# Three small moves at the start of a fused attention, MLP and soft-routing kernel: a side product, one load, one scan

## The reference, cut to what matters

```
# 1: recurrent attention, batch 4, 8 heads, 768 steps, head size 48
for t in range(768):
    y[t]  = r[t] @ (state + (u * k[t]) v[t]^T)
    state = w[t] * state + k[t] v[t]^T
# 2: MLP, 3072 tokens, 384 -> 2048 -> 384
h = x @ w_in;  g = h * clip(h + 3, 0, 6) / 6;  x = g @ w_out
# 3: soft routing, 32 slots (8 experts of 4), 3072 tokens
logits = x @ phi
d = softmax over tokens;  slots = d^T x;  slots = relu(slots @ w1[e]) @ w2[e]
out = softmax over slots(logits) @ slots
```

## Time and profile before

| | us |
|---|---|
| time, median of 3 runs (lowest, highest) | 431.91 (431.82, 432.13) |
| the profiled execution's own time | 432.12 |
| its span, first to last instruction | 430.4 |
| PE busy | 410.6 (95%) |
| DVE busy | 333.8 (78%) |
| POOL busy | 196.4 (46%) |
| ACT busy | 155.4 (36%) |

### The profile page before, as it was taken

One profiled execution on the slowest core, in us unless ns is written; L12 is line 12 of the kernel. 1 busy time (PEld: TensorE's weight loads), 2 busy tenths in 40 slices (PEclk: granted clock), 3 DMA queues, 4 the chain that ended last, 5 costly groups with the idle time before them and its releaser, 6 DMA issues.

```text
span 430.4 us, 9672 instructions
## 1 busy us (share of the span) xinstructions
PE 410.6 (95%) x3898; PEld 222.6 (52%) x3898; DVE 333.8 (78%) x535; ACT 155.4 (36%) x263; POOL 196.4 (46%) x183
## 2 busy tenths in 40 slices
PE   8999899999999999999999999989999999999981
PEld 3875555556555555555565555455554443433430
DVE  7798799998988989889889889898866687641142
ACT  2265355533334244144342342432333234211142
POOL 7747888874645663455654456634630012010000
PEclk9999999999999999999999999999999999999996
DMA  8996312468034223403440332131008961589829
GB/s 248 354 392 250 121 60 63 121 244 283 17 111 121 72 55 116 123 0 121 121 121 2 121 119 86 44 113 56 2 0 339 404 216 70 225 319 423 354 83 357
DMA packets 15245, 69.35 MB, mean 161 GB/s; under 512 B 2016, under 2 KB 2656, under 8 KB 13152
## 3 DMA queue, kind: packets, MB, share of 16 engines
q1 hardware_dynamic: 15200, 68.73, 45.0%
HBM read 64.00 MB, written 4.72 MB: 160 GB/s over the span
## 4 chain that ended last, share of the span: by engine, by line
PE 74%; DVE 8%; issue 6%; DMA 5%; POOL 3%; ACT 2%; SPq 0%; POOLq 0%; DVEq 0%
PE hid L544 13%; PE hid L546 12%; PE hid L545 12%; PE l_ps L579 5%; PE y_ps L510 5%; PE l_ps L611 4%; PE sc_ps L445 4%; DMA att<-rkT_dram 3%; PE hid L757 2%; PE inc_ps L470 2%; PE y_ps L527 2%; DVE att L817 2%; PE sc_ps L611 1%; PE hid L738 1%; PE sc_ps L738 1%
## 5 line engine op out<-in xcount | busy, mean ns | idle before, releaser
L1184 ACT ACTIVATE relu<-hid,three 128x512 f32<-128x512 f32 x96 | 65.9, 687 | 141.7 <-PE hid L546 140.9
L544 PE MATMUL hid<-x_split,w_split 128*128 128x512 f16 x288 | 109.4, 380 | 0.0
L546 PE MATMUL hid<-x_split,w_split 128*128 128x512 f16 x288 | 109.1, 379 | 0.0
L545 PE MATMUL hid<-x_split,w_split 128*128 128x512 f16 x288 | 109.1, 379 | 0.0
L904 DVE SCALAR_TENSOR_TENSOR gated<-relu,hid 128x512 f32<-128x512 f32 x96 | 65.1, 679 | 28.3 <-ACT relu L1184 27.7
L914 DVE STREAM_TRANSPOSE ring<-gated 128x512 f32<-128x512 f32 x96 | 68.3, 711 | 3.3
L1332 POOL TENSOR_TENSOR att<-att 128x1024 f16<-128x1024 f32 x20 | 40.5, 2026 | 50.6 <-ACT att L1129 50.6
L1350 POOL TENSOR_TENSOR att<-att 112x512 f32<-112x512 f32 x19 | 22.4, 1181 | 58.7 <-DVE att L829 58.7
L544 PEld LDWEIGHTS hid<-x_split,w_split 128*128 128x128 f16 x288 | 28.2, 98 | 37.5 <-issue 8.6
L546 PEld LDWEIGHTS hid<-x_split,w_split 128*128 128x128 f16 x288 | 28.1, 98 | 34.0
L545 PEld LDWEIGHTS hid<-x_split,w_split 128*128 128x128 f16 x288 | 28.2, 98 | 25.1 <-issue 0.3
(11 more groups left out here) (228 smaller groups left out, 752.5 us busy)
## 6 DMA issues: line engine op xcount, KB each, us to landing
att<-nat_dram SPq DMA_DIRECT2D x20, 576.0 KB, 4.1
att<-rkT_dram SPq DMA_DIRECT2D x22, 448.0 KB, 5.5
att<-w_dram SPq DMA_DIRECT2D x5, 1536.0 KB, 14.2
att<-wT_dram SPq DMA_DIRECT2D x22, 226.2 KB, 4.8
out_dram<-w_split SPq DMA_DIRECT2D x12, 384.0 KB, 3.9
stage<-w_in_dram SPq DMA_DIRECT2D x2, 1536.0 KB, 13.5
ring<-w_outT_dram SPq DMA_DIRECT2D x1, 3072.0 KB, 15.7
stage<-w_dram SPq DMA_DIRECT2D x2, 1536.0 KB, 9.9
```

The lines of the kernel that those rows point to most:

```text
L544: pe.matmul(hid[s % 2][:], high, x_high, start=(q == 0), stop=False)
L545: pe.matmul(hid[s % 2][:], high, x_low, start=False, stop=False)
L546: last = pe.matmul(hid[s % 2][:], low, x_high, start=False, stop=(q == KT - 1))
L1184: nc.scalar.activation(relu_tile(s), hid[s % 2][:], ACT.Relu, bias=three[:], scale=GATE / H_SCALE)\
```

## The change

Four edits. The load of w_outT is issued in front of the load of unit 4's r, k and v rows (`load_nat(4)`). In unit 3 two of the three parts of w_out times phi replace three `stay_warm` matmuls, two ahead of `attend_first(3)` and one behind it; the third part takes the place of the first in MLP step 0, and the parts in steps 1 and 2 are gone. On DVE the low half of piece 1 goes behind the prefix scan of unit 5 (the sixth unit), and the transpose into w_phi goes from step 4 to step 1.

```diff
             sp.dma_start(u_all, u.rearrange("h d -> (h d)").partition_broadcast(P)).then_inc(u_in, 16)
+            sp.dma_start(w_outT_stage, w_outT).then_inc(w_outT_in, 16)
             load_nat(B)
-            sp.dma_start(w_outT_stage, w_outT).then_inc(w_outT_in, 16)
             load_rows(B + 1)
...
                     turn_keys(n)
-                stay_warm(2, hid[0])
+                if n + 1 < B:
+                    stay_warm(2, hid[0])
+                else:
+                    weigh_phi(0)
                 attend_first(n)
                 if n + 1 < B:
                     diagonal(n + 1)
-                stay_warm(1, hid[0])
+                    stay_warm(1, hid[0])
+                else:
+                    weigh_phi(1)
                 turn_x(n)
...
                 if s == 0:
                     turn_keys(B)
-                    weigh_phi(0)
+                    weigh_phi(2)
...
                     if n == B + 1:
                         attend(B)
-                        weigh_phi(1)
...
-                if s == 2:
-                    weigh_phi(2)
...
                 if s == 0:
-                    low_w(1)
                     sum_diag(B)
                 if phase == 3:
                     if is_unit(n + 1):
                         scan_prefix(n + 1)
+                    if s == 0:
+                        low_w(1)
...
-                if s == 4:
+                if s == 1:
                     dve.wait_ge(w_phi_ready, 4)
                     nc.vector.transpose(w_phi[:], l_ps[:]).then_inc(w_phi_done, 1)
```

## The result

The changed kernel takes 433.45 us (median of 20 runs, 431.80 to 437.25), the kernel before 431.95 (20 runs, 431.78 to 432.24): ratio 1.0036, 95% interval 1.0022 to 1.0051. It is slower, and outside the range of the prediction (430.7 to 432.7). More than the median, the spread has changed. Of the 20 runs 13 are over 432.77, the bound for a slower kernel; of before, none. The fastest runs of both are equal. In the changed kernel the runs with the long times mostly have the lower mean granted clock: 0.983 to 0.987 in the five over 435, 0.990 to 0.994 in the six under 432.4. (The mean alone doesn't mark a long run: the kernel before also has runs of 431.88 us at 0.985; where that can come from is said at the end of the experiments.)

The account below looks back on a forecast made before the run. The DVE/POOL hand-over sets the pace up to about 85 us, then PE. Net gain 0.35 us: profiled 432.12 becomes 431.77, which lies 0.21 above the median, so forecast 431.55 us; range 430.7 to 432.7.

Parts of the forecast that it names:

- the paragraph on PE: PE from unit 3 on: added groups cost 0 and 0.18 us; dropping those of steps 1 and 2 frees 2.0 us.
- near 1.5: Sign of being right: PE's wait ahead of unit 5's scores is longer than 1.08 us, near 1.5.
- The load: w_outT, issued at about 12.3, lands at 31.1 us (bounds 30.6 and 32.5), before the first group at 31.38.
- Rival 2: w_outT lands late, delaying PE's first group in unit 3; landing at 32.5 gives 432.65 us; chance 0.13.
- Unit 3: PE's two weigh_phi groups in unit 3: the first costs 0, the second 0.18 us, bounds 0.1 and 0.25.
- DVE and POOL: Around step 0, pieces sharing SBUF ports run in one row; unit 5's scores start at 47.13 for 47.57, gaining 0.44 us.
- the four pieces: Scan, diag_values(4), low_w(1) and decay_receptance(5) on DVE and POOL, in that order, ending at 44.55, 45.17, 45.98 and 47.03.
- the order at `low_w(2)`: POOL's low_w(2) goes ahead of DVE's suffix scan of unit 6, taking about 1.6 us instead of 2.58.
- The transpose into w_phi: On DVE it adds 0.61 to 0.69 us, so the mask starts at 49.0; leaving step 4 gives nothing.
- Carrying through: Gains in the first 60 us reach the end if DVE and POOL get earlier; 0.3 to 0.45 us, 0.35 taken.

Follow-up runs that it names:

- the last version: Changed kernel with low_w(1) behind gate(1) and its transpose, the transpose into w_phi back in step 4, three f16 fillers behind attend(4): 431.23 us, ratio 0.9984.
- groups-left-out: Changed kernel with unit 3's f16 fillers back and groups 0 and 1 omitted, group 2 alone making w_phi: 432.00 us, ratio 1.0021, 4 of 12 runs long.

## Why the prediction was wrong

**The step that failed** is in the paragraph on PE: the group of step 1 "stood ahead of the 1.08 us wait for POOL and only makes that wait longer". I priced that at zero, since PE waits for POOL either way. It isn't: the wait went to 1.67 us, and 20 of 31 runs became long, by 0.9 to 5.3 us over 431.95. In the one long run of this kernel that was profiled the clock falls behind this wait, and so it does in the long profiles of two of its variants; with the wait filled or cut to 1.0 us the long runs are gone. I had even forecast the gap ("near 1.5") as a sign that I was right. The group in the gap did two things: besides its result it kept PE at work, and three fillers in its place do that as well (432.09). I looked for clock trouble nowhere, because the trace of before had full clock until PE's last matmul, and that trace is of a kernel whose gap at this place is 1.08 us. The gap of 1.64 us at 287.59 in the same trace would have said that such a gap is harmless, too.

**The load.** Right in the main: it landed at 30.8 (30.6 to 31.4 was named), with no wait in the three profiles of the changed kernel and nothing late behind it. But the 0.3 us in hand is thin: in the last version's profile it landed at 31.7 and PE waited 0.34 us. Rival 2 had half of the truth: a late load costs what it is late and the half clock on top (3.6 us of wait, 7 us in the end). But the long runs of the changed kernel are not that: they stay when groups 0 and 1 don't need the load, and they go with fillers in the gap while the load stays.

**Unit 3.** Mis-sized: 0.35 us against 0.18, and outside the bounds of 0.1 and 0.25. The start of the y group moves by 0.05 us (2.57 to 2.62 us behind the start of unit 3's scores), the step from there to the second group takes 0.12 us more than that to the filler did (34.24 - 32.33 against 34.20 - 32.41), and the second group costs the 0.18. Why the y group takes longer no run shows.

**DVE and POOL.** The mechanism was right, the order wrong. Each held the other up (the Trainium skill, SBUF — State Buffer, Who interferes with whom, calls the shared ports an exclusive lock, and the rows agree). But low_w(1) came directly behind the scan and ahead of POOL, which had been waiting for 1.1 us (43.48 to 44.53); I had let the waiting one in first. By the page's rule the one that issues first gets the ports, which would have been POOL's diag_values; here the rows differ from it, and they decide. So low_w(1) took 0.93 us and not 1.4, diag_values 2.66 and not 1.7, decay_receptance its normal 1.17. The sum of the four pieces is nearly the same whatever their order; they took 0.2 us more than I had added up, a few hundredths at each hand-over. So the order brought 0.42 us and not 0.62 (the 0.44 of the forecast and the 0.18 that unit 3 was to cost). gate(1) came 0.25 us earlier (0.12 counted from unit 3's scores) rather than 0.28 later, so the order at `low_w(2)` did not turn either (2.57 and 1.42 us as before). With low_w(1) apart from the scan, diag_values took the 1.75 us that I had expected.

**The transpose into w_phi.** In step 1 it filled DVE's wait ahead of the mask (0.73 us before). The mask starts at 48.64, not at 49.0 as forecast, so the transpose cost nothing there. That step 4 gives nothing back is as forecast: DVE's wait for POOL ahead of `finish_y` grew from 0.20 to 0.81 us.

**Carrying through.** Right: with the scan first and nothing else the scores come 0.42 us sooner and the median is 0.5 us lower. But the sum was too small even without the clock's part: 0.42 for the order less 0.35 for unit 3 leaves 0.06 or 0.07 us, not 0.35. The forecast of 431.55 would still have been 0.4 us too low: the kernel with the gap filled has 431.99.

**What stays open.** The start of the low clock differs: by the clock of the 2 us stretches 0.4 us ahead of the scores (46.4), 0.25 behind their start (47.4) and 1.1 behind it (48.8). So does its length (3.4 us twice, 6.8 us in the groups-left-out profile). The profiles don't show what makes one run fall and the next not, nor why the gap of 1.64 us near 288 us has no fall behind it in any of them and the shorter one near 415 us sometimes has. The simplest test of the place was not run either: the kernel before with only the group of step 1 taken out. Nor is it shown why the same gap of 1.66 us gave 9 long runs of 12 with groups in unit 3 and 4 of 12 with fillers; with so few runs it can be chance. In the last version the move of low_w(1) and that of the transpose were not run apart.

## What to carry to other kernels

That another engine sets the end of an idle gap of PE doesn't make the gap free: work that is taken out in front of a wait lengthens it, and here 0.6 us more of it turned a steady kernel into one that loses 1 to 5 us in most of its runs. So move work out of a gap only if the gap that it leaves stays short, or leave a filler there, and time both, since another gap of the same length did no harm. Where two profiles agree but the runs spread, look at the granted clock of a long run, stretch by stretch and not in the mean, before reasoning on from a short one. And compare two profiles from an event ahead of the change, not by their clock times.

## What the runs showed of the hardware

TensorE's clock fell from 2.4 to 1.2 GHz (granted clock 1.00 to 0.50) around or behind an idle gap of 1.65 or 1.66 us in three profiles (433.72, 433.18 and 434.74 us), with 1.00 in every stretch from 31 us to the gap. It stayed at half for 3.4, 3.4 and 6.8 us, while PE worked without a pause from the scores on. In a wait of 3.63 us it fell 1.8 us after the wait began and was full again only at 43.2, 8.4 us after PE had gone on.

The same length does not always do it: behind 1.64 or 1.65 us near 288 us the clock stayed full in all fourteen profiles, and behind 1.28 us near 415 it fell in three of them.

A DVE instruction with two SBUF inputs that follows directly on another one kept POOL out through both: 2.66 us for an instruction that took 0.83 us at 60.29 in the same profile, and 1.69 behind one scan. With a gate and a transpose between the two, POOL got in (1.75 us).
